# Attention feeding an expert layer on one core: later transposes, inverse sums by way of DRAM, scores in three reduced-precision products

## What is computed

```python
q_pool = q.reshape(B, H, S // 2, 2, D).mean(axis=3)
scores = np.matmul(q_pool, k.transpose(0, 1, 3, 2)) / np.sqrt(D)
scores = scores - np.max(scores, axis=-1, keepdims=True)
attn = np.exp(scores)
attn = attn / (np.sum(attn, axis=-1, keepdims=True) + 1e-09)
x = np.matmul(attn, v).transpose(0, 2, 1, 3).reshape(B * S // 2, H * D)
h = x @ w_in
g = np.maximum(h, 0.0) + alpha * np.minimum(h, 0.0)
out = g @ w_out
```

## Time and profile before

| | before |
|---|---|
| median of 3 runs | 931.14 us (930.97 to 931.58) |
| the profiled execution's own time | 932.26 us |
| its span | 929.7 us |
| mean granted clock of PE | 0.998 |
| PE busy | 887.3 us, 95% |
| PEld busy | 623.2 us, 67% |
| DVE busy | 516.9 us, 56% |
| ACT busy | 423.4 us, 46% |
| POOL busy | 213.3 us, 23% |
| DMA | 79.57 MB, mean 86 GB/s |

### The profile page before, as it was taken

One profiled execution on the slowest core, in us unless ns is written; L12 is line 12 of the kernel. 1 busy time (PEld: TensorE's weight loads), 2 busy tenths in 40 slices (PEclk: granted clock), 3 DMA queues, 4 the chain that ended last, 5 costly groups with the idle time before them and its releaser, 6 DMA issues. The chain is left out here.

```text
span 929.7 us, 20770 instructions
## 1 busy us (share of the span) xinstructions
PE 887.3 (95%) x6896; PEld 623.2 (67%) x6896; DVE 516.9 (56%) x836; ACT 423.4 (46%) x963; POOL 213.3 (23%) x182
## 2 busy tenths in 40 slices
PE   3799999999999999999999999999999999999997
PEld 1455555555555555555545799989999999989995
DVE  2676767677767776767676344344444444343442
ACT  2566666666666666666666222222322222322222
POOL 2112111211121112111200323323232323323230
PEclk9999999999999999999999999999999999999999
DMA  7435423542354235523520122212422222322211
GB/s 186 106 83 135 119 65 82 133 121 63 82 133 123 60 82 133 127 57 82 133 71 1 59 68 58 67 62 63 136 57 68 57 68 61 132 59 66 65 36 68
DMA packets 36366, 79.57 MB, mean 86 GB/s; under 512 B 5360, under 2 KB 9456, under 8 KB 36336
## 3 DMA queue, kind: packets, MB, share of 16 engines
q1 hardware_dynamic: 33936, 74.48, 31.0%
q10 hardware_dynamic: 2400, 4.72, 1.5%
HBM read 74.46 MB, written 4.72 MB: 85 GB/s over the span
## 5 line engine op out<-in xcount | busy, mean ns | idle before, releaser
L432 DVE TENSOR_REDUCE neg_max<-s_ps 128x1 f32<-128x1152 f32 x144 | 194.1, 1348 | 16.6 <-DVEq L431 16.6
L573 PE MATMUL pv_ps<-pt,v_f 128*64 128x256 f32 (+1 forms) x1152 | 169.0, 414 | 0.0
L532 PE MATMUL s_ps<-k_f,q_f 64*128 64x512 f32 (+1 forms) x640 | 160.2, 626 | 5.2 <-PEq L543 5.2
L348 ACT ACTIVATE e_sb<-s_ps,neg_max 128x1024 f32<-128x1024 f32 x144 | 160.1, 1112 | 0.0
L587 PEld LDWEIGHTS slot_ps<-ident,e_sb 64*128 64x128 f32 x2304 | 86.0, 139 | 82.4 <-issue 82.4
L465 DVE COPY pt<-slot_ps 128x512 f32<-128x512 f32 x144 | 99.6, 692 | 61.3 <-DVEq L464 59.4
L341 ACT ACTIVATE e_sb<-s_ps,neg_max 128x128 f32<-128x128 f32 x144 | 52.9, 367 | 171.5 <-ACTq L340 171.5
L617 PE MATMUL slot_ps<-x_hi,wi_hi 128*128 128x384 f32 x384 | 129.5, 337 | 1.1 <-PEq L613 1.1
L617 PE MATMUL slot_ps<-x_lo,wi_hi 128*128 128x384 f32 x384 | 129.5, 337 | 0.0
L617 PE MATMUL slot_ps<-x_hi,wi_lo 128*128 128x384 f32 x384 | 129.0, 336 | 0.0
L479 DVE TENSOR_SCALAR e_sb<-slot_ps,alpha_sb 128x384 f32<-128x384 f32 x96 | 59.3, 618 | 123.2 <-DVEq L477 123.2
(11 more groups left out here) (46 smaller groups left out, 1098.8 us busy)
## 6 DMA issues: line engine op xcount, KB each, us to landing
q_raw<-in_q SPq DMA_DIRECT2D x64, 288.0 KB, 4.5
k_f<-in_k SPq DMA_DIRECT2D x64, 288.0 KB, 4.2
wi_raw<-in_w_in SPq DMA_DIRECT2D x48, 256.0 KB, 2.6
wo_raw<-in_w_out SPq DMA_DIRECT2D x48, 256.0 KB, 2.6
v_f<-in_v SPq DMA_DIRECT2D x32, 288.0 KB, 3.0
out<-pt ACTq DMA_DIRECT2D x6, 768.0 KB, 4.4
k_end<-in_k SPq DMA_DIRECT2D x64, 32.0 KB, 4.0
alpha_sb<-in_alpha SPq DMA_DIRECT2D x1, 8.0 KB, 4.7
```

Of the source, the lines that this page charges most:

```text
L348: nc.scalar.activation(e_sb[:, b * NKEY + at:b * NKEY + at + n], s_ps[:, S_AT[b] + at:S_AT[b] + at + n], ACT.Exp, bias=neg_max[:, b:b + 1] ...
L432: nc.vector.tensor_reduce(out=neg_max[:, b:b + 1], in_=s_ps[:, S_AT[b]:S_AT[b] + NKEY], op=ALU.max, axis=AX_X, negate=True).then_inc(max_r ...
L532: ins = nc.tensor.matmul(s_ps[to:to + m, S_AT[b] + at:S_AT[b] + at + BANK], q_f[2 * g + h][rows, first:first + m], k_f[2 * g + h][rows, at ...
L573: ins = nc.tensor.matmul(pv_ps[h * D:(h + 1) * D, 0:n], v_f[2 * g + h][:, a, :], pt[:, a, at:at + n], start=(a == 0), stop=(a == KT - 1))
```

## The change

Five parts, each in the code below.

1. **Lag.** PE transposes tile s-1 in step s (before: tile s), and waits for `exp_done` behind these transposes, ahead of the scores of s+2. `e_sb` has three buffers. `PRODUCT`, `invert` (now t = 5 and t = 0) and `scale` (now t = 1 and t = 6) stand one step later; one more step closes the attention.
2. **Inverse sums.** `spread_inverse` and ACT's copies of it go. SP waits for `invert`, stores each tile's 128 sums to a row in DRAM (six DMAs for group 0, four for group 1), waits until they have landed, and reads the row back, repeated over 64 partitions, with two DMAs. `scale` waits for these.
3. **Scores.** q and k are split into high and low fp32r parts, and `big_scores` does three fp32r products (high q by high k, high q by low k, low q by high k) for each of its two pieces of 512 keys. In MIX the weights of both heads are 128 wide, with zeros in the other head's columns (q has 64 zero columns twice for that, so 640 columns), so it is six products for each piece.
4. **Splitting q and k.** k goes to one buffer `k_raw`; POOL makes the high and low parts and copies the two key ends into `k_end`, whose own DMAs go. `k_raw` and `q_raw` are each one buffer for all heads, freed by POOL. The first heads' parts are made by DVE and ACT.
5. **x.** `scale` writes x whole (`x_f`). Its two parts are made a pass at a time, in the memory that the parts of q and k had: the first by POOL during the last pair, the others by ACT and DVE in the last body of the pass before.

```diff
-    PRODUCT = {5: (0, (0, 1)), 6: (0, (2, 3)), 7: (0, (4, 5)), 8: (0, (6, 7, 8)),
-               0: (1, (0, 1)), 1: (1, (2, 3)), 2: (1, (4, 5)), 3: (1, (6, 7)), 4: (1, (8,))}
-    SPREAD = {6: 0, 1: 1}
-    INVERT = {4: 0, 8: 1}
-    FIRST = 6
+    PRODUCT = {6: (0, (0, 1)), 7: (0, (2, 3)), 8: (0, (4, 5)), 0: (0, (6, 7, 8)),
+               1: (1, (0, 1)), 2: (1, (2, 3)), 3: (1, (4, 5)), 4: (1, (6, 7)), 5: (1, (8,))}
+    INVERT = {5: 0, 0: 1}
+    SCALE = {1: 0, 6: 1}
+    FIRST = 7
...
+            def load_qk(head):
+                sp.wait_ge(q_raw_free, 1).then_inc(q_raw_free, -1)
+                load_q(head, q_raw, q_raw_in)
+                sp.wait_ge(k_raw_free, 1).then_inc(k_raw_free, -1)
+                load_k(head, k_raw, k_raw_in)
...
+            def spread(group):
+                a, b = GROUP_TILES[group]
+                at, other, n, first = GROUPS[group]
+                whole = [t for t in range(a, b) if t != MIX]
+                sp.wait_ge(inv_ready, 1).then_inc(inv_ready, -1)
+                for i in range(0, len(whole), 2):
+                    for h in range(2):
+                        to = GROUPS[group][h] + i // 2 * P
+                        t = whole[i + h]
+                        sp.dma_start(sums[to:to + P], inv_sum[:, t:t + 1]).then_inc(inv_stored, 16)
...
+                stores = len(whole) + (2 if group == 0 else 0)
+                sp.wait_ge(inv_stored, 16 * stores).then_inc(inv_stored, -16 * stores)
+                for h in range(2):
+                    row = sums[GROUPS[group][h]:GROUPS[group][h] + n]
+                    sp.dma_start(inv_bc[h * D:(h + 1) * D, first:first + n],
+                                 row.rearrange("(o n) -> o n", o=1).to_broadcast([D, n])).then_inc(inv_bc_in[group], 16)
...
+            load_q(0, q_raw, q_first_in[0]), load_k(0, k_raw, k_first_in[0])
+            load_k(1, k_raw1, k_first_in[1]), load_q(1, q_raw1, q_first_in[1])
+            load_qk(2), load_qk(3)
             load_v(0, 0), load_v(1, 1)
...
+            with sp.Fori(0, NPAIR // 2 - 2) as two:
+                for g in range(2):
+                    spread(0)
+                    load_v_pair(two * 2 + 2 + g, g)
+                    load_qk_pair(two * 2 + 3 + g)
+                    spread(1)
...
+            def split_q(i, raw, done):
+                pool.wait_ge(done, 32).then_inc(done, -32)
+                nc.gpsimd.tensor_tensor(raw[:, 0, :], raw[:, 0, :], raw[:, 1, :], ALU.add).then_inc(pool_self, 1)
...
+                nc.gpsimd.tensor_copy(q_hi[i], q_f[i][:, :]).then_inc(pool_self, 1)
...
+                nc.gpsimd.tensor_tensor(q_lo[i], q_f[i][:, :], q_hi[i].bitcast(F32), ...
...
+            def split_qk(i):
+                split_q(i, q_raw, q_raw_in)
                 pool.sem_inc(q_raw_free, 1)
+                pool.wait_ge(k_raw_in, 32).then_inc(k_raw_in, -32)
+                nc.gpsimd.tensor_copy(k_hi[i], k_raw[:, :]).then_inc(pool_self, 1)
...
+                nc.gpsimd.tensor_tensor(k_lo[i], k_raw[:, :], k_hi[i].bitcast(F32), ALU.subtract).then_inc(pool_self, 1)
...
+                nc.gpsimd.tensor_copy(k_end[i][0:D, :, :], key_ends(k_raw[0:D, :])).then_inc(pool_self, 1)
...
+                pool.sem_inc(k_ready[i], 1)
+                pool.sem_inc(k_raw_free, 1)
+            def split_pair(g):
+                pool.wait_ge(qk_free[g], 1).then_inc(qk_free[g], -1)
+                split_qk(2 * g), split_qk(2 * g + 1)
...
+                if t in SCALE and pair is not None:
+                    scale(SCALE[t], pair + (0 if s < 2 * TILES else 1))
+                    if SCALE[t] == 1:
+                        dve.sem_inc(v_free[1 - g], 1)
+                if s > 0:
+                    dve.wait_ge(tr_ready[1], 1).then_inc(tr_ready[1], -1)
+                    nc.vector.tensor_copy(pt_half((s - 1) % TILES, 1), ...
...
+                for j, (qp, kp, col) in enumerate(terms):
+                    for row, at in enumerate(BIG[b]):
+                        rows = slice(row * HALF, (row + 1) * HALF)
+                        pieces[row] = nc.tensor.matmul(s_ps[:, S_AT[b] + at:S_AT[b] + at + BANK],
+                                                       qp[rows, col:col + P], kp[rows, at:at + BANK],
+                                                       start=(j == 0), stop=(j == len(terms) - 1))
...
             def step(s, pair, left=2):
...
+                if s > 0:
                     for i in range(2):
+                        pe.wait_ge(slot_free[i], 1).then_inc(slot_free[i], -1)
+                    for a in range(2 * CH):
+                        at = (s - 1) % 3 * NKEY + a * P
...
+                if left >= 0:
+                    pe.wait_ge(exp_done, 1).then_inc(exp_done, -1)
                 if left > 1:
                     begin_scores(s + 2)
```

More of the change, by code:

```diff
@@ L13, with build @@
 BANK = 512
-def build(nc, q, k, v, w_in, w_out, alpha, out):
+def build(nc, q, k, v, w_in, w_out, alpha, sums, out):
     HEADS, D, NKEY = k.shape
-    NQ = q.shape[3]
+    NQ = NKEY // 2
+    QCOLS = q.shape[3]
     FT, DM = w_out.shape[0], w_out.shape[2]
@@ L124, in build @@
         q_ready = [sem(f"q{i}_ready") for i in range(4)]
+        k_ready = [sem(f"k{i}_ready") for i in range(4)]
+        k_hi_done = sem("k_hi_done")
+        k_raw_read = sem("k_raw_read")
         pool_self = sem("pool_self")
@@ L178, in over_steps, with key_ends, x_chunk, x_part @@
                     step(s, two * 2)
-            for s in range(FIRST, REST):
+            for s in range(FIRST, REST + 1):
                 step(s, 2 * BODIES, REST - 1 - s)
+        def key_ends(keys):
+            return keys.rearrange("p (a c) -> p a c", c=P)[:, 0:KT:KT - 1, :]
+        def x_chunk(n, h):
+            at = (2 * n + h) * TOK
+            return x_f[:, :].rearrange("p (d c) -> p d c", d=DT)[:, :, at:at + TOK]
+        def x_part(part, h):
+            return part[h].rearrange("p (d c) -> p d c", d=DT)
         def pt_half(t, half):
@@ L202, in _, with load_q @@
         def _(sp):
[L203 to L211, removed]
-                sp.dma_start(k_end[i][0:D, 0, :], k[head, :, 0:P]).then_inc(k_in[i], 16)
-                sp.dma_start(k_end[i][0:D, 1, :], k[head, :, NKEY - P:NKEY]).then_inc(k_in[i], 16)
+            def load_q(head, to, done):
+                sp.dma_start(to[0:D, :, :], q[head, :, :, :]).then_inc(done, 16)
+                sp.dma_start(to[D:P, :, :], q[head, :, :, :]).then_inc(done, 16)
@@ L403, in hidden @@
                     act.wait_ge(g_ready, 1).then_inc(g_ready, -1)
-                    nc.scalar.activation(g_hi[0][:, :], g_sb, ACT.Copy).then_inc(g_hi_done, 1)
+                    nc.scalar.activation(g_hi[0], g_sb, ACT.Copy).then_inc(g_hi_done, 1)
+                    if last and not last_pass:
+                        x_high(n + 1, 0)
                     if first:
@@ L414, in hidden @@
                     act.wait_ge(g_ready, 1).then_inc(g_ready, -1)
-                    nc.scalar.activation(g_hi[1][:, :], g_sb, ACT.Copy).then_inc(g_hi_done, 1)
+                    nc.scalar.activation(g_hi[1], g_sb, ACT.Copy).then_inc(g_hi_done, 1)
+                    if last and not last_pass:
+                        x_high(n + 1, 1)
                     if not (last_pass and isinstance(f, int) and f >= FT - 2):
@@ L507, in hidden @@
                     if n == 0 and not first:
-                        scale(1)
-                        x_high(NPAIR - 1)
+                        scale(1, NPAIR - 1)
+                    if last and not last_pass:
+                        x_low(0)
                     unit(f, 1)
+                    if last and not last_pass:
+                        x_low(1)
                 over_hidden(dve, hidden)
@@ L603, in step, with hidden_unit @@
                 group, tiles = PRODUCT[t]
-                if group == 0 or pair is not None:
-                    if t in SPREAD:
-                        pe.wait_ge(slot_free[0], 1).then_inc(slot_free[0], -1)
-                        spread_inverse(SPREAD[t], slot_ps[0])
-                    product(group, g if group == 0 else 1 - g, tiles)
-            def hidden_unit(n, f, i, h):
+                if t > 5:
+                    product(group, g, tiles)
+                elif pair is not None:
+                    product(group, 1 - g, tiles)
+            def hidden_unit(n, f, i, h, first):
+                if not first:
+                    pe.wait_ge(x_ready, 1).then_inc(x_ready, -1)
                 if h == 0:
```

331 lines of the change are left out of this document (177 added, 154 removed).

## The result

The changed kernel takes 1104.43 us (1102.50 to 1106.15, four runs) against 931.2 us (930.97 to 931.58) of the kernel before: a ratio of 1.186, interval 1.184 to 1.188. I had forecast 920 us, 884 to 950, and faster. It is 173 us slower.

What follows compares the result with a forecast made beforehand. PE bounds the kernel before; after the change SP's queue round, 30.4 us a pair against PE's 27.2, was to bound it. 932.26 - 13.4 (earlier expert layer) + 2 (x's parts) = 920.9 profiled, 920 us as median; range 884 to 950.

Steps and rivals of the forecast that it cites:

- SP and POOL, a pair: SP's DMA queue followed once round: 30.4 us against PE's 27.2, so SP's round sets the attention pair.
- the landing of the 4-byte stores: Inverse sums stored to DRAM by SP: 2.6 us from issue to landing, with bounds 1.5 and 4.7.
- POOL, first head: POOL's splitting of the first head's q and k within SP's round: 10.2 us, until `k_raw` is free.
- SP's round is longer: Rival, chance 0.25: the two 4-byte store landings in SP's queue take longer; 946 or 975 us in its examples.
- The whole: Sum over startup, thirteen SP rounds, end and expert layer: expert layer starts at about 502.5 us, total 920 us.
- small-write rule: SP's stores to DRAM: writes below 512 bytes are read, modify and write, making the round longer; no size given.
- PE, a pair: PE's work per attention pair falls from 30.90 to 27.2 us: 1.36 inverse sums, 1.38 scores, 0.96 transpose waits.
- The point on row halves: PE's large scores: fp32r products on the two row halves run side by side, 0.81 us a step, MIX 1.50.
- one after the other: Rival, chance 0.06: PE's row-half score products run serially, 1.50 us a step, MIX 2.88; pair 34.1, time 983 us.
- steps outside 6 and 7 wait for exponentials: Stated sign, in PE's attention steps, that the prediction is wrong; no size given.
- the lag: PE in each attention step: transposing before waiting for the newest exponentials removes 0.96 us of waits a pair.
- DVE waits before `scale` in t = 6: Expected sign in the attention: DVE waits 2 to 3 us a pair for the row, PE a step later.

Runs made afterwards that it cites:

- the single store: Changed kernel with only the first of each group's six or four stores of inverse sums done, read-back from w_in instead; 1052.4 us.
- the kernel with PE's inverse sums: Changed kernel with its second part undone, so the inverse sums go through PE and ACT again; 948.3 us, ratio 1.018.
- the kernel of 915.4 us: Changed kernel, small stores collected in an SBUF row written to DRAM whole, loads issued between stores and reads, invert's addition with one operand; 915.4 us, ratio 0.983.

## Why the prediction was wrong

**The step that failed** is in the first and the last item of "SP and POOL, a pair": the landing of the 4-byte stores. I priced it at 2.6 us, the weight load with as many pieces, between 1.5 and 4.7. The round by its terms, forecast and measured (332.25 is where the reads of 331.14 end, and the round before gives POOL's part):

| term | forecast | measured |
|---|---|---|
| six stores, landing, two reads | 5.95 | 10.97 (332.25 to 343.22) |
| v and q, to POOL's start | 7.95 | 8.9 (301.44 to 310.35) |
| POOL, first head | 10.2 | 10.8 (310.35 to 321.19) |
| k of the second head | 1.2 | 1.1 |
| four stores, landing | 3.8 | 8.8 (322.31 to 331.14) |
| two reads | 1.3 | 1.1 |
| round | 30.4 | 41.8 |

10.0 of the 11.4 us are the two landings. Taken from the start of the last store, the landing is some 7 us, outside the bounds that I had drawn from loads: none of my rows was a store to DRAM. Pieces set apart land in 1.9 us by the DMA view, inside my bounds. The rival "SP's round is longer" had the mechanism, the place and the rule of its price right (12 to 13 times what it adds) and the chance of 0.25; with 41.8 it would have said 920 + 13 x 11.4 = 1068.

Of the rivals after the result, the number of stores is out by the single store, and the load of the memory by the pieces set apart, which land quickly under the same loads. The place of the waits in SP's order is real (68 to 79 us), but doesn't make a landing quick. The other parts of the change leave 17 us net, by the 948.3 us of the kernel with PE's inverse sums.

The whole, by the start of the expert layer, 682.55 for my 502.5, 180.0 us late. The group 0 read-back of pair 1 was to be issued at 68.9 + 4.75 = 73.7 and came at 92.00: 18.3, since in the startup too every landing is waited for. Thirteen rounds: 635.84 - 92.00 = 543.8 for 395.2, 148.6. The end: 46.7 for 33.6, 13.1; I had said that the wait goes there, and it doesn't. The expert layer takes 418.2 us (1100.7 - 682.55), 4.3 more than before, where I had added 2.

The landing wasn't the only error. With pieces apart, landing inside my bounds, the time of 955.1 is still above my range. By the same sum its 35 us over 920 are 2.6 in the startup (read-back of pair 1 at 76.23), 21.9 in thirteen rounds of 32.1 us (to 493.35), 9.1 behind them (expert layer at 536.11) and 1.4 in the expert layer. In one such round (303.16 to 334.78) POOL's first head is 0.65 us above my term and the four stores behind k, with their landing, 0.8; the other terms are within 0.2. (My terms for POOL's head add up to 10.1, not 10.2.)

**The page's rule.** Beside the sum I had the small-write rule of the Trainium skill, "DMA: Bandwidth & Descriptors", section "Specifications", by which the round would be longer. The sign agrees, but the rule doesn't make the difference: the pieces set 64 bytes apart are as far below 512 bytes each and land in 1.9 us.

**PE, a pair.** Forecast 27.2 us; where SP doesn't bound it is 29.2 to 29.3 us (253.28 to 341.10 are three pairs of the kernel of 915.4 us). The point on row halves held: the products run side by side, six records in 0.95 us and MIX in 1.64, so that the rival "one after the other" is out. But the terms were 0.81 and 1.50. From 8 x (0.95 - 0.81) + 0.14 come 1.3 us by these durations, which overlap with their neighbours; by the pitch to the ninth piece (343.10 to 344.01 in the changed kernel, 0.91) it is 0.9. The rest is what I had named as a way to be wrong: steps outside 6 and 7 wait for exponentials. The ninth piece goes every 3.10 us from step 3 to step 6 (271.43, 274.53, 277.63, 280.73), each time behind a wait. A chain comes round once a step: small scores on PE, row maximum on DVE (1.35 us), exponential of the small part on ACT (0.37 us), for which PE waits before it writes the ninth piece and the next small scores. By these rows it, and not PE's work, sets the 3.10 us; no run with less work on PE was made to show it. I had priced the lag as if nothing but the transposes depended on the exponentials.

**Other steps.** DVE waits before `scale` in t = 6, as I said, but it is 5.1 to 18.3 us, not 2 to 3, and PE waits in that same step for the accumulator. POOL's copies are cheap, as I took them, 0.77 us for q and 1.14 for k; q has 704 columns, not 640 (its subtraction 1.67 us for 1.5). DVE was not next as an engine, as I said (though its busy time, 346.5 / 16 = 21.7 us a pair less 0.45 for the cast, is 78% of 27.2, not near 70%), but I didn't ask what POOL's work, which goes from 84.2 us to 283.2 in the attention, does to an instruction of DVE beside it. Clock: I left it at its full level; behind each of the 14 waits of step 6 the product takes 2.40 us instead of 1.30, as at the lower level.

## What to carry to other kernels

Price a DMA by a row that goes in the same direction and has the same shape at its destination; a load says nothing of many 4-byte writes side by side in DRAM. Where a value must go from partitions to a row, collect the pieces in SBUF and write DRAM in one piece, and give the queue something to issue meanwhile: that order gained 79 us with quick landings and 68 with late ones, which hold the loads up as well. Where POOL's work grows, list the short DVE instructions with two SBUF operands on the chain to the row maximum, and give them one operand.

## What was not expected of the hardware

A DMA of 128 pieces of 4 bytes, side by side in DRAM, lands after 7.8 us; 32 pieces 4.9, 16 pieces 2.0; the same 128 pieces 64 or 512 bytes apart 1.9, and side by side in SBUF 2.1. In the one other order that was tried, neighbours in the store 64 bytes apart, they were no quicker. What distance is enough below 64 bytes wasn't tried. While it is under way, a load issued behind it is held up too (13.4 us from q's issue to POOL, for 6.9 in the changed kernel and 6.1 with quick stores in the same order). What is done with the pieces side by side, why 16 pieces are still quick, and whether the loads are held in the queue or in the memory stays open; no run here separates them.

An addition of five columns on DVE, with two operands in SBUF, took 2.23 us beside a running POOL instruction of 2.65 us and ended with it. POOL's instruction need not have two operands: beside a copy of one the addition of four columns took 0.73 us, in the kernel with PE's inverse sums:

```profile
149.26 0.77 POOL L325 CAST kq<-q_f 128x704 fp32r<-128x704 f32 x1 [0.17 <-POOLq L324]
149.32 0.73 DVE L524 SCALAR_TENSOR_TENSOR sum_eps<-row_sum 128x4 f32<-128x4 f32 x1
```

With one operand it took 0.16 beside a POOL addition of two, as here in the kernel of 915.4 us:

```profile
319.63 1.68 POOL L380 TENSOR_TENSOR q_raw<-q_raw 128x704 f32<-128x704 f32 x1 [6.33 <-POOLq L379]
319.68 0.16 DVE L575 TENSOR_REDUCE sum_eps<-row_sum 128x4 f32<-128x8 f32 x1
```
